# Attention, routed experts and a domain mixture on one core: routing work, meta scatters and first loads put in another order

## The chip, the cores and the metric

The kernel runs on one core of one Trainium2 chip. The metric is the device time of one execution in microseconds (us), as the median of several runs. A profiled execution of the kernel before gives the trace; its clock starts at the first instruction of the program, and all times below count from there. The engines are TensorE (PE, with its weight loads as PEld), VectorE (DVE), ScalarE (ACT), GpSimd (POOL) and SyncE (SP), which only issues transfers. A name with a q behind it (PEldq, SPq) is the engine's own sequencer: register loads, branches and issues of transfers.

## The reference

Three stages in float32, on 2 x 576 = 1152 tokens of 512 features:

```python
# attention: 8 heads of 64; heads 0-3 see the last 32 positions, heads 4-7 every 32nd position
scores = scale * q @ k.T            # masked, softmax, then @ v
x = attn_out.transpose(0, 2, 1, 3).reshape(1152, 512)

# routed experts: one of 8 per token
logits = x @ w_gate + modality_bias[modality_id]
e_idx = argmax(logits, 1); gate_w = softmax(logits)[n, e_idx]
for e in range(8):
    out[mask_e] = gate_w[mask_e, None] * (relu(x[mask_e] @ w1[e]) @ w2[e])   # 512 -> 1024 -> 512

# mixture of 4 domains: every token through every domain
p = domain_probs / domain_probs.sum(-1)
for e in range(4):
    out += p[:, e:e+1] * (relu(x @ u1[e]) @ u2[e])
```

## The kernel before, in words

Every engine has its own program, written out by hand, and they meet at semaphores. There is no planner: the order of the instructions in each program is the order of the work, and a wait stops all that stands behind it on that engine.

**Attention** (TensorE from line 1258, VectorE from 862, ScalarE from 583, GpSimd from 468, all over the same step number i). There are STEPS = 22 blocks of queries, 11 for each of the 2 batches (5 of the strided heads, then 6 of 96 rows of the local heads). In step i TensorE makes the scores of block i, transposes the probabilities of block i - 3 and multiplies block i - 5 with v; VectorE finds row maxima and reciprocal sums and copies results to xT; ScalarE does the exponentials; GpSimd multiplies with the reciprocal (line 471). When enough blocks are done, a token tile (128 tokens, NT = 9 of them) is flipped to rows (flip_rows) and kept in xtok by ScalarE (even tiles) or VectorE (odd tiles), and its 8 logits are computed (gate_logits).

**Routing** is done in three groups of three token tiles. find_experts (line 795) makes the one-hot choice of a group, rank_group on TensorE (1245) counts the tokens before each one, find_slots (814) turns that into a row number in the buffer x_by_expert in device memory, in which each expert has a range of rows. After the first group, at CHOSEN_AT = block 13 (step 18), choose_first (821) picks the expert with the most tokens so far, so that its weights and its first two tiles can be worked on before all is known. put_in_order (831) gives its start rows x_first (columns 0 and 1: first and second tile, 3: the tail to be filled with zeros) and the order of the other experts; find_bases (849) prepares the table of tiles. All three are small instructions on VectorE inside attention steps: choose_first in step 18, put_in_order and the find_slots of the first group in step 19, find_bases in step 20.

**Scatter** (465). GpSimd writes each token tile's rows to x_by_expert with one indirect transfer per tile. The first tile is scattered behind the product of step 20, the second and third after the loop, the other six when the first expert tile has been loaded (xt_in) and their slots are known.

**SyncE's queue** (from 336) is one list: inputs; w1 of the first expert once first_known; a zero fill behind the expert's rows; the first tile x_tile (375) once the fill and the first three scatters have landed; w2 of that expert (376); fill and second tile (381, 385); eight more fills (389); the third tile (394); then a loop that loads w1 and w2 of the other experts; last the sorted meta rows (409).

**Expert tiles.** Float32 products are made of three products of parts in float32r (hi x hi, hi x lo, lo x hi). ScalarE rounds the high part (cut_w1, cut_w2, keep_xt, keep_ht), VectorE subtracts for the low part (split_w1, split_w2, keep_xt, keep_ht). One tile on TensorE (whole_tile, 1382): 24 matmuls of 128x512 with w1 in two halves, flips of h, x and y between them, 24 matmuls with w2. w1 comes in four chunks; the first expert's are cut and split in steps W1_AT = 23 to 26 of the attention loop. Tiles 0 and 1 are written out (1392 to 1409), the others run in a loop whose bounds each engine loads from the table (1412 to 1416 on TensorE, 1097 to 1105 on VectorE). The table comes from count_tiles, find_offsets, make_table and place_tiles on VectorE (984 to 1060), and signals table_ready.

**Meta.** find_meta (1062) gives each token its rank in the sorted order, and a row with its number, and its gate weight times the four domain probabilities. Nine indirect transfers of GpSimd (489), one per token tile, sort these rows into meta_by_rank; the mixture reads them. After them GpSimd waits for the y of the third tile and loads and splits the first domain weights.

**Mixture** (from 1421). All tokens, sorted, go through the four domains; half of the steps use a seven-product scheme for 2x2 blocks. Results are added up in acc and scattered to out. The diff does not touch it.

Of the kernel before, what the change touches and what calls it, by code (L numbers as in the profile page):

```python
# [22 lines left out]
ALU = mybir.AluOpType  # L23
# [17 lines left out]
def moe_chain(nc, qT_in, kT_in, v_in_pos, v_in_res, modality_id, w_gate, modality_bias, w1, w2, domain_probs, u1, u2, out):  # L41
# [65 lines left out]
    W1_AT = [STEPS + LAG_V - 4 + c for c in range(4)]  # L107
# [40 lines left out]
    with ctx:  # L148
# [188 lines left out]
        def _(sp):  # L337
# [12 lines left out]
            for b in range(B):  # L350
                if b == 1:
                    sp.wait_ge(kT_zeroed_g, 1)
                for kind, tiles in ((0, range(STRIDED)), (1, range(STRIDED, TILES))):
                    load_qk(b, kind)
                    for n in tiles:
# [12 lines left out]
            sp.wait_ge(x_first_known, 1)  # L368
# [7 lines left out]
            sp.dma_start(w2_raw[:].unsqueeze(1),  # L376
                         w2[bass.ds(expert, 1)].rearrange("e (c p) d -> p e c d", p=P)).then_inc(w2_in, 16)
# [7 lines left out]
            sp.dma_start(x_tile[:], xb[bass.ds(x1, P), :]).then_inc(xt_in, 16)  # L385
            sp.wait_ge(rest_known, 1)
# [3 lines left out]
            sp.wait_ge(x2_known, 1)  # L390
            x2 = sp.value_load(x_first[0:1, 2:3], min_val=0, max_val=(E - 1) * ROWS + 2 * P)
            sp.wait_ge(filled, 16 * E)
            sp.wait_ge(xt_flipped, 2)
            sp.dma_start(x_tile[:], xb[bass.ds(x2, P), :]).then_inc(xt_in, 16)
# [18 lines left out]
        def _(pool):  # L413
# [54 lines left out]
            for i in range(STEPS):  # L468
                R, C, s = rows(i % TILES), keys(i % TILES), i % PB
                pool.wait_ge(inv_known, i + 1)  # L470
                g.tensor_tensor(prob[0:R, s, :, 0:C], prob[0:R, s, :, 0:C],
                                row_inv[0:R, s, :].unsqueeze(2).to_broadcast([R, HALF_H, C]),
                                ALU.mult).then_inc(normed, 1)
                if i == STEPS - 2:
                    pool.wait_ge(slot_ready, 1)
                    pool.wait_ge(x_kept_a, 2)
                    pool.wait_ge(x_kept_v, 1)
                    scatter(0)
            for t in range(1, NT):
                for g_, (t0, t1) in enumerate(GROUPS):  # L480
                    if t == t0:
                        pool.wait_ge(xt_in, 16)
                        pool.wait_ge(slot_ready, g_ + 1)
                        pool.wait_ge(x_kept_a, (t1 + 1) // 2)
                        pool.wait_ge(x_kept_v, t1 // 2)
                scatter(t)
            pool.wait_ge(meta_ready, 3)
            for t in range(NT):
                pool.indirect_dma_start(out=ms, out_offset=bass.IndirectOffsetOnAxis(ap=pos[:, t:t + 1], axis=0),
                                        in_=meta[:, t, :], in_offset=None).then_inc(meta_scattered, 16)  # L490
            pool.wait_ge(scattered, 16 * (NT - GROUPS[0][1]))
# [48 lines left out]
            pool.wait_ge(y_kept, 3)  # L540
# [3 lines left out]
            split_u2(0)  # L544

# [27 lines left out]
        def _(act):  # L573
# [62 lines left out]
            for t in FLIP_END:  # L636
                if t % 2 == 0:
                    keep_rows(t)
            act.wait_ge(w2_in, 16)
# [16 lines left out]
            keep_xt(2)  # L656
            act.wait_ge(table_ready, 1)
            act.wait_ge(filled, 16 * E)
            load_x(3)
            keep_ht(1, 1)  # L660
# [91 lines left out]
        def _(dve):  # L752
# [37 lines left out]
            def step(ins):  # L790

                ins.then_inc(vstep, 1)
                dve.wait_ge(vstep, st.next())
# [27 lines left out]
            def choose_first():  # L821

                dve.wait_ge(vstep, st.value)
                step(w.reduce_max(choice[:, 0:1], count_a[:], axis=AX.X))
                step(w.scalar_tensor_tensor(out=early_n[:], in0=count_a[:], scalar=choice[:, 0:1], in1=e_down[:],
                                            op0=ALU.is_ge, op1=ALU.mult))
                step(w.reduce_max(choice[:, 1:2], early_n[:], axis=AX.X))
                w.tensor_scalar(first_expert[:], choice[:, 1:2], -1.0, float(E), ALU.mult, ALU.add).then_inc(first_known, 1)
                step(w.tensor_scalar(is_e0[:], e_down[:], choice[:, 1:2], None, ALU.is_equal))

            def put_in_order():
# [4 lines left out]
                w.tensor_copy(x_first[:, 0:1], choice[:, 2:3]).then_inc(vstep, 1)  # L836
                st.next()
                w.tensor_tensor(x_first[:, 3:4], choice[:, 2:3], choice[:, 0:1], ALU.add).then_inc(vstep, 1)
                st.next()
                step(w.tensor_tensor(x_first[:, 1:2], choice[:, 2:3], choice[:, 3:4], ALU.add))  # L840
                w.tensor_scalar(at_least[:], is_e0[:], float(EARLY), None, ALU.mult).then_inc(x_first_known, 1)
# [20 lines left out]
            for i in range(STEPS + LAG_V):  # L862
# [60 lines left out]
                if m == CHOSEN_AT + 1:  # L923
                    put_in_order()
                    find_slots(slice(*GROUPS[0]))
                if m == CHOSEN_AT + 2:
                    find_bases()
# [15 lines left out]
            keep_xt(0)  # L943
            dve.wait_ge(logit_done, 1)
# [149 lines left out]
            keep_y(1)  # L1094
# [3 lines left out]
            n_runs = dve.value_load(table[0:1, 4, 0:1], min_val=1, max_val=E)  # L1098
            with dve.Fori(0, n_runs) as r:
# [126 lines left out]
        def _(pe):  # L1226
# [174 lines left out]
            x_w1(0, 0, 0, range(DC)).then_inc(h_done, 1)  # L1401
            rank_last()
            x_w1(0, 0, 1, range(DC // 2))
# [150 lines left out]
```

## Time and profile before

| what | value |
|---|---|
| median of 3 runs | 650.02 us (649.83 to 651.19) |
| the profiled execution's own time | 652.64 us |
| its span, first to last instruction | 650.9 us |
| TensorE busy | 614.7 us, 94% |
| VectorE / ScalarE / GpSimd busy | 55% / 32% / 46% |
| mean granted clock of TensorE | 0.967 |
| chain that ended last: TensorE | 84% |
| chain: VectorE / issue / transfers / ScalarE / unknown queue | 6% / 4% / 2% / 1% / 1% |

The page cuts the span in 40 slices of 16.3 us. TensorE's granted clock, in tenths, is 9 (full) in all of them but the six slices from 49 to 146 us, where it is 8, 5, 8, 7, 8 and 7. Attention runs to about 76 us, the expert tiles from 81 to 265 us, the mixture from there to the end. How to read it: busy shares are averages over stages with different limits, so what an edit is worth is read from the chain and the waits of the stage it lies in. Ends of matmuls are modelled. In a timeline row the columns are start, duration, engine, line, operation, output and inputs, and in brackets how long the engine had been idle and what released it. A chain row has start, duration and the engine and line that the end of the program waited for at that time.

### The profile page before, as it was taken

Reading aid. Unit: us, or ns where it says so; the run is one execution under the profiler, and the core shown is the slowest. Engines: PE = TensorE matmul, PEld = TensorE weight load, DVE = VectorE, ACT = ScalarE, POOL = GpSimd, SP = SyncE. Lnnn points to the kernel's source line nnn. Section 1 sums busy time; section 2 is a strip of 40 time slices with the busy share of each in tenths; the row PEclk is TensorE's granted clock in tenths of the full one; section 3 lists DMA queues with packets and bytes.
Section 4 is the critical chain, followed back from the end, with each engine's and each line's share of the span. In section 5 each row is a group of like instructions: output and inputs, shape, how many; then the busy total and the mean of one; then the engine's idle time right before and its main releaser. Section 6 shows DMA issues by size and latency. Waiting matters only on the chain.

```text
span 650.9 us, 10557 instructions
## 1 busy us (share of the span) xinstructions
PE 614.7 (94%) x3604; PEld 536.9 (82%) x3605; DVE 358.5 (55%) x735; ACT 207.7 (32%) x528; POOL 299.6 (46%) x278
## 2 busy tenths in 40 slices
PE   5998988969999999999999999999999999999995
PEld 4887966758666688989989988988998998998894
DVE  4877655212788722359555455556545545545553
ACT  3865332212777423204213212311321321231230
POOL 6534230335000000571999685485576568547005
PEclk9998587879999999999999999999999999999999
DMA  9904533723478400100122201110110110110003
GB/s 234 230 3 157 201 125 134 277 52 109 161 274 281 139 16 16 49 33 1 64 65 66 65 33 33 66 51 14 64 64 5 59 64 32 32 64 0 0 0 146
DMA packets 27091, 56.68 MB, mean 87 GB/s; under 512 B 6840, under 2 KB 9528, under 8 KB 27064
## 3 DMA queue, kind: packets, MB, share of 16 engines
q1 hardware_dynamic: 18632, 31.93, 15.4%
q0 software_dynamic: 6848, 21.52, 9.7%
q10 hardware_dynamic: 1584, 2.88, 1.6%
q8 instruction: 15, 0.25, 0.2%
q14 instruction: 12, 0.10, 0.1%
HBM read 48.97 MB, written 7.36 MB: 87 GB/s over the span
## 4 chain that ended last, share of the span: by engine, by line
PE 84%; DVE 6%; issue 4%; DMA 2%; ACT 1%; another core or an unknown queue 1%; POOL 1%; ACTq 0%; SPq 0%; DVEq 0%; POOLq 0%
PE bank L1456 30%; PE bank L1427 28%; PE bank L1351 9%; PE bank L1363 6%; PE bank L1276 2%; PE bank L1242 2%; PE bank L1313 1%; DVE w_lo L859 1%; PE bank L1341 1%; PE bank L1237 1%; PE bank L1286 1%; DMA kT<-in_kT 1%; PE bank L1335 1%; PE bank L1271 1%
## 5 line engine op out<-in xcount | busy, mean ns | idle before, releaser
L1148 DVE SCALAR_TENSOR_TENSOR acc<-bank,meta_s,acc 128x512 f32<-128x512 f32 x135 | 100.8, 749 | 63.3 <-PE bank L1456 63.2
L1456 PE MATMUL bank<-u_hi,h_hi 128*128 128x512 f32 x288 | 112.3, 390 | 0.0
L1456 PE MATMUL bank<-u_lo,h_hi 128*128 128x512 f32 x288 | 112.1, 389 | 0.0
L1456 PE MATMUL bank<-u_hi,h_lo 128*128 128x512 f32 x288 | 112.0, 389 | 0.0
L516 POOL CAST u_hi<-u_raw 128x1792 fp32r<-128x1792 f32 (+1 forms) x16 | 25.6, 1600 | 112.3 <-PE bank L1427 110.0
L1195 DVE SCALAR_TENSOR_TENSOR h_lo<-bank,h_hi 128x288 fp32r<-128x288 f32 x112 | 51.0, 455 | 44.7 <-ACT h_hi L728 22.9
L1427 PE MATMUL bank<-x2T_hi,u_hi 128*128 128x288 f32 x232 | 68.4, 295 | 0.0
L1427 PE MATMUL bank<-x2T_lo,u_hi 128*128 128x288 f32 x232 | 68.4, 295 | 0.0
L1427 PE MATMUL bank<-x2T_hi,u_lo 128*128 128x288 f32 x232 | 68.3, 295 | 0.0
L1427 PE MATMUL bank<-t_hi,u_hi 128*128 128x288 f32 x224 | 66.2, 295 | 0.0
L1427 PE MATMUL bank<-t_lo,u_hi 128*128 128x288 f32 x224 | 66.0, 295 | 0.0
L1427 PE MATMUL bank<-t_hi,u_lo 128*128 128x288 f32 x224 | 65.9, 294 | 0.0
L1456 PEld LDWEIGHTS bank<-u_hi,h_lo 128*128 128x128 f32 x288 | 54.1, 188 | 11.4
L1456 PEld LDWEIGHTS bank<-u_hi,h_hi 128*128 128x128 f32 x288 | 54.0, 188 | 10.2
L1456 PEld LDWEIGHTS bank<-u_lo,h_hi 128*128 128x128 f32 x288 | 54.1, 188 | 10.1
L518 POOL TENSOR_TENSOR u_lo<-u_raw,u_hi 128x1792 fp32r<-128x1792 f32 (+1 forms) x16 | 61.6, 3850 | 1.3
L716 ACT COPY part_p<-bank 128x288 f32<-128x288 f32 x28 | 11.2, 401 | 157.9 <-PE bank L1427 157.9
L508 POOL TENSOR_TENSOR u_raw<-u_raw 128x256 f32<-128x256 f32 x14 | 10.3, 736 | 88.1 <-PE bank L1427 71.4
L1351 PE MATMUL bank<-w_hi,xt_hi 128*128 128x512 f32 x96 | 42.5, 443 | 4.7 <-DVE w_lo L859 3.0
L1427 PEld LDWEIGHTS bank<-x2T_hi,u_hi 128*128 128x128 f32 x232 | 43.5, 188 | 0.7
L1427 PEld LDWEIGHTS bank<-x2T_lo,u_hi 128*128 128x128 f32 x232 | 43.5, 188 | 0.6
L1427 PEld LDWEIGHTS bank<-x2T_hi,u_lo 128*128 128x128 f32 x232 | 43.5, 188 | 0.0
(226 smaller groups left out, 1258.8 us busy)
## 6 DMA issues: line engine op xcount, KB each, us to landing
w_raw<-in_moe_w SPq DMA_DIRECT2D x10, 2048.0 KB, 8.9
u_raw<-in_moe_w POOLq DMA_DIRECT2D x16, 512.0 KB, 3.7
u_raw<-in_moe_w POOLq DMA_DIRECT2D x16, 256.0 KB, 3.1
u_raw<-in_moe_w POOLq DMA_DIRECT2D x32, 128.0 KB, 2.9
x_tile<-x_by_expert ACTq DMA_DIRECT2D x11, 256.0 KB
x_by_expert<-zero_row SPq DMA_DIRECT2D x10, 256.0 KB, 2.0
qT<-in_qT SPq DMA_DIRECT2D x4, 576.0 KB, 8.4
kT<-in_kT SPq DMA_DIRECT2D x8, 288.0 KB, 9.7
```

The lines of the kernel that those rows point to most:

```text
L508: g.tensor_tensor(u1_raw[:, S1], u1_raw[:, A21], u1_raw[:, A22], ALU.add).then_inc(u_summed, 1)
L516: g.tensor_copy(u1_hi[n % 2][:, need], u1_raw[:, need]).then_inc(u1_hi_cut, 1)
L518: g.tensor_tensor(u1_lo[n % 2][:, need], u1_raw[:, need], u1_hi[n % 2][:, need].bitcast(FP32), ALU.subtract)\
L716: a.copy(part[s][k][:], bank[s][:, 0:SUB]).then_inc(part_kept[s], 1)
L1148: w.scalar_tensor_tensor(out=acc[:, t, :], in0=bank[Z_BANK[i]][:], scalar=meta_s[:, t, bass.ds(e + 1, 1)], in1=acc[:, t, :], op0=ALU.mult, ...
L1195: w.scalar_tensor_tensor(out=h_lo[:, i, cols_of(s, k)], in0=bank[at][:, 0:SUB], scalar=0.0, in1=h_hi[:, i, cols_of(s, k)].bitcast(FP32), o ...
L1242: last = t_.matmul(where, xT[:, c, P * t:P * (t + 1)], gate[:, c, :], start=c == 0, stop=c == DC - 1)
L1276: last = t_.matmul(bank_s[0:R, h, 0:C], qT[:, b, c, q0:q0 + R], kT[:, b, c, h % 2, k0:k0 + C], start=False, stop=True, skip_group_check=True)
L1351: last = t_.matmul(bank[half][:], lhs[:, c, :], rhs[:, c, fs], start=c == 0 and i == 0, stop=c == DC - 1 and i == 2)
L1363: last = t_.matmul(bank[5][:], lhs[:, f, :], rhs[:, f, :], start=f == 0 and rhs is w2_hi and lhs is ht_hi, stop=f == FCH - 1 and lhs is ht_lo)
L1427: last = t_.matmul(bank[at][:, 0:SUB], lhs_part[page][:, lhs, c, :], rhs[:, c, :], start=start and c == 0 and i == 0, stop=c == KC - 1 and ...
L1456: last = t_.matmul(bank[Z_BANK[i]][:], lhs[:, c, ts], rhs[page][:, c, :], start=c == 0 and k == 0, stop=c == 1 and k == 2)
```

## The change

- **Spread.** The rows x_first are made by a new function place_first, one attention step after choose_first; find_slots of the first group comes one step later than before (step 20), the rest of put_in_order in step 21, find_bases in step 22.
- **Scatters.** The first three scatters are issued behind the products of steps 19, 20 and 21.
- **First loads.** SyncE issues the w2 load as soon as x_first is known, before the zero fill and the first tile. The third tile's load is put before the eight fills and no longer waits for them.
- **w1 chunks.** Three chunks are cut and split in steps 24 to 26; the fourth after the loop (ScalarE: behind its last row copy; VectorE: behind keep_xt(0), ahead of the last logits). TensorE's rank_last moves between the third and the fourth chunk of the first product.
- **Waits before the loop.** ScalarE does keep_ht(1, 1) before it waits for the table and the fills. VectorE does keep_y(1) after find_meta and after its loads of n_tiles and n_runs.
- **Meta.** The scatter of meta block t waits for y of tile t; the first three stand before the loads and splits of the first domain weights, the other six behind them.

```diff
-    W1_AT = [STEPS + LAG_V - 4 + c for c in range(4)]
+    SCATTER_FROM = STEPS - GROUPS[0][1]
+    W1_AT = [STEPS + LAG_V - 3 + c for c in range(3)]
```

On SyncE:

```diff
-            sp.wait_ge(x_first_known, 1)
+            sp.wait_ge(x_first_known, 3)
+            sp.dma_start(w2_raw[:].unsqueeze(1),
+                         w2[bass.ds(expert, 1)].rearrange("e (c p) d -> p e c d", p=P)).then_inc(w2_in, 16)
             x0 = sp.value_load(x_first[0:1, 0:1], min_val=0, max_val=(E - 1) * ROWS)
...
             sp.dma_start(x_tile[:], xb[bass.ds(x0, P), :]).then_inc(xt_in, 16)
-            sp.dma_start(w2_raw[:].unsqueeze(1),
-                         w2[bass.ds(expert, 1)].rearrange("e (c p) d -> p e c d", p=P)).then_inc(w2_in, 16)
...
+            sp.wait_ge(x2_known, 1)
+            x2 = sp.value_load(x_first[0:1, 2:3], min_val=0, max_val=(E - 1) * ROWS + 2 * P)
+            sp.wait_ge(xt_flipped, 2)
+            sp.dma_start(x_tile[:], xb[bass.ds(x2, P), :]).then_inc(xt_in, 16)
             sp.wait_ge(rest_known, 1)
             for e in range(E):
                 tail = sp.value_load(fill_rest[0:1, e:e + 1], min_val=0, max_val=E * ROWS)
                 sp.dma_start(xb[bass.ds(tail, P), :], zero_row[:]).then_inc(filled, 16)
-            sp.wait_ge(x2_known, 1)
-            x2 = sp.value_load(x_first[0:1, 2:3], min_val=0, max_val=(E - 1) * ROWS + 2 * P)
-            sp.wait_ge(filled, 16 * E)
-            sp.wait_ge(xt_flipped, 2)
-            sp.dma_start(x_tile[:], xb[bass.ds(x2, P), :]).then_inc(xt_in, 16)
```

On GpSimd (the issue of one meta block is as before):

```diff
-                if i == STEPS - 2:
+                if i == SCATTER_FROM:
                     pool.wait_ge(slot_ready, 1)
                     pool.wait_ge(x_kept_a, 2)
                     pool.wait_ge(x_kept_v, 1)
-                    scatter(0)
-            for t in range(1, NT):
+                if i >= SCATTER_FROM:
+                    scatter(i - SCATTER_FROM)
+            for t in range(GROUPS[0][1], NT):
...
-            pool.wait_ge(meta_ready, 3)
-            for t in range(NT):
+            def scatter_meta(t):
+                pool.wait_ge(y_kept, t + 1)
                 pool.indirect_dma_start(out=ms, out_offset=bass.IndirectOffsetOnAxis(ap=pos[:, t:t + 1], axis=0),
...
-            pool.wait_ge(y_kept, 3)
+            pool.wait_ge(meta_ready, 3)
+            for t in range(3):
+                scatter_meta(t)
             load_u1(0)
             load_u2(0)
             split_u1(0)
             split_u2(0)
+            for t in range(3, NT):
+                scatter_meta(t)
```

On ScalarE:

```diff
                     keep_rows(t)
+            cut_w1(WCH - 1)
             act.wait_ge(w2_in, 16)
...
             keep_xt(2)
+            keep_ht(1, 1)
             act.wait_ge(table_ready, 1)
             act.wait_ge(filled, 16 * E)
             load_x(3)
-            keep_ht(1, 1)
```

On VectorE:

```diff
+            def place_first():

                 w.tensor_scalar(choice[:, 2:3], choice[:, 1:2], -float(ROWS), float(E * ROWS), ALU.mult, ALU.add).then_inc(vstep, 1)
                 st.next()
                 step(w.tensor_scalar(choice[:, 3:4], choice[:, 0:1], float(P), None, ALU.min))
-                w.tensor_copy(x_first[:, 0:1], choice[:, 2:3]).then_inc(vstep, 1)
+                w.tensor_copy(x_first[:, 0:1], choice[:, 2:3]).then_inc(x_first_known, 1)
+                w.tensor_tensor(x_first[:, 3:4], choice[:, 2:3], choice[:, 0:1], ALU.add).then_inc(x_first_known, 1)
+                w.tensor_tensor(x_first[:, 1:2], choice[:, 2:3], choice[:, 3:4], ALU.add).then_inc(x_first_known, 1)
+
             def put_in_order():
+                step(w.tensor_scalar(is_e0[:], e_down[:], choice[:, 1:2], None, ALU.is_equal))
...
                 if m == CHOSEN_AT + 1:
+                    place_first()
+                if m == CHOSEN_AT + 2:
+                    find_slots(slice(*GROUPS[0]))
+                if m == CHOSEN_AT + 3:
                     put_in_order()
-                    find_slots(slice(*GROUPS[0]))
-                if m == CHOSEN_AT + 2:
+                if m == CHOSEN_AT + 4:
                     find_bases()
...
             keep_xt(0)
+            split_w1(0, WCH - 1)
             dve.wait_ge(logit_done, 1)
...
-            keep_y(1)
             find_meta()
             dve.wait_ge(table_ready, 1)
             n_tiles = dve.value_load(table[0:1, 4, 1:2], min_val=EARLY + 1, max_val=MAXT)
             n_runs = dve.value_load(table[0:1, 4, 0:1], min_val=1, max_val=E)
+            keep_y(1)
```

On TensorE:

```diff
-            x_w1(0, 0, 0, range(DC)).then_inc(h_done, 1)
+            x_w1(0, 0, 0, range(DC - 1))
             rank_last()
+            x_w1(0, 0, 0, range(DC - 1, DC)).then_inc(h_done, 1)
```

## Rows read from the trace of the kernel before

**Rows 1.** Timeline of TensorE: start, us, engine, line, operation, idle before

```profile
60.32 0.55 PE L1286 MATMUL bank<-ident,prob 96*128 96x96 f32 x4 [2.19 <-POOL prob L471]
...
115.18 1.48 PE L1363 MATMUL bank<-w_hi,ht_hi 128*128 128x512 f32 x4 [2.45 <-ACT ht_hi L623]
...
136.05 2.08 PE L1363 MATMUL bank<-w_hi,ht_hi 128*128 128x512 f32 x4 [5.70 <-ACT ht_hi L623]
```

**Rows 2.** Timelines of VectorE and ScalarE, routing work and the end of attention

```profile
55.65 0.16 DVE L833 TENSOR_SCALAR choice<-choice 128x1 f32<-128x1 f32 x1
...
57.91 0.17 DVE L819 CAST slot<-slot_f 128x3 uint32<-128x3 f32 x1
...
80.11 0.17 DVE L946 TENSOR_TENSOR logits<-bank,bias_tok 128x16 f32<-128x16 f32 x1 [1.56 <-PE bank L1242]
...
81.18 0.18 DVE L805 TENSOR_TENSOR onehot<-r,first 128x24 bf16<-128x24 f32 x1
...
81.53 1.99 ACT L611 CAST w_hi<-w_raw 128x1024 fp32r<-128x1024 f32 x2
...
86.03 0.18 DVE L810 TENSOR_TENSOR rank_e<-bank,e_rows 128x24 f32<-128x24 f32 x1 [4.52 <-PE bank L1249]
...
113.08 0.68 DVE L938 TENSOR_TENSOR xt_lo<-bank,xt_hi 128x512 fp32r<-128x512 f32 x1
```

**Rows 3.** Windows: length, busy PE, PEld, DVE, ACT, POOL, PEclk, DMA share, GB/s

```profile
61.30:85.00 23.70, 22.61 (x122) 20.72 (x121) 12.73 (x39) 10.00 (x19) 8.10 (x8) 0.50 0.54 196
...
115.90:119.30 3.40, 3.40 (x10) 2.62 (x9) 0.00 (x0) 0.00 (x0) 0.00 (x0) 0.50 0.97 344
...
132.90:139.80 6.90, 3.75 (x9) 2.98 (x10) 0.69 (x1) 0.59 (x1) 0.67 (x1) 0.51 0.01 1
```

**Rows 4.** Chain of waits in order of time: start, us, what was waited for

```profile
76.00 0.85 PE bank L1329 x4
...
81.02 4.75 PE bank L1351 x12
...
94.95 2.51 DMA x_tile<-x_by_expert
...
99.56 5.49 PE bank L1351 x12
...
119.78 2.74 PE bank L1351 x12
...
128.10 7.29 another core or an unknown queue
...
140.81 2.75 PE bank L1351 x12
...
153.62 2.72 PE bank L1351 x12
```

**Rows 5.** Timeline of SyncE's queue, the first expert's loads

```profile
54.96 0.39 SPq L366 DMA_DIRECT2D w_raw<-in_moe_w  x1
...
58.03 0.38 SPq L372 DMA_DIRECT2D x_by_expert<-zero_row  x1
...
69.67 0.36 SPq L375 DMA_DIRECT2D x_tile<-x_by_expert  x1
```

**Rows 6.** Two weight loads in a row: window 114 to 129, queue 1 from 122.4

```profile
114.00:129.00 15.00, 13.72 (x60) 10.99 (x60) 4.11 (x13) 3.47 (x6) 4.96 (x6) 0.89 0.81 298
...
q1 hardware_dynamic: 763, 1.58, 103.2%
```

**Rows 7.** Register loads from the table on TensorE and VectorE, by line

```profile
L1412 PEldq TENSOR_LOAD <-table x1: 488/488/488, 115.9 to 115.9; - x1
...
L1100 DVEq TENSOR_LOAD <-table x5: 302/307/324, 123.7 to 213.1; - x5
L1097 DVEq TENSOR_LOAD <-table x1: 553/553/553, 122.0 to 122.0; - x1
```

**Rows 8.** Transfers into meta_by_rank: ns min, median, max, first and last start

```profile
L489 POOL DMA_INDIRECT meta_by_rank<-meta,pos x9: 952/957/961, 122.5 to 132.6; - x9
```

More of the change, by code:

```diff
@@ L828, in choose_first @@
                 w.tensor_scalar(first_expert[:], choice[:, 1:2], -1.0, float(E), ALU.mult, ALU.add).then_inc(first_known, 1)
-                step(w.tensor_scalar(is_e0[:], e_down[:], choice[:, 1:2], None, ALU.is_equal))
-            def put_in_order():
+            def place_first():
                 w.tensor_scalar(choice[:, 2:3], choice[:, 1:2], -float(ROWS), float(E * ROWS), ALU.mult, ALU.add).then_inc(vstep, 1)
@@ L835, in put_in_order @@
                 step(w.tensor_scalar(choice[:, 3:4], choice[:, 0:1], float(P), None, ALU.min))
-                w.tensor_copy(x_first[:, 0:1], choice[:, 2:3]).then_inc(vstep, 1)
+                w.tensor_copy(x_first[:, 0:1], choice[:, 2:3]).then_inc(x_first_known, 1)
+                w.tensor_tensor(x_first[:, 3:4], choice[:, 2:3], choice[:, 0:1], ALU.add).then_inc(x_first_known, 1)
+                w.tensor_tensor(x_first[:, 1:2], choice[:, 2:3], choice[:, 3:4], ALU.add).then_inc(x_first_known, 1)
+            def put_in_order():
+                step(w.tensor_scalar(is_e0[:], e_down[:], choice[:, 1:2], None, ALU.is_equal))
+                w.tensor_scalar(at_least[:], is_e0[:], float(EARLY), None, ALU.mult).then_inc(vstep, 1)
                 st.next()
[L838 to L841, printed above, removed]
                 w.tensor_scalar(early_n[:], is_e0[:], choice[:, 3:4], None, ALU.mult).then_inc(vstep, 1)
```

## Prediction

> **What bounds the kernel now.** I read the granted clock by stretch first, then the chain of waits in order of time from 45 to 170 us, then the timelines of the engines where that chain leaves TensorE. From 139.8 us on the chain is TensorE's almost alone and the page's clock line shows full speed; the diff touches nothing there except some of the meta scatters. So the change can only win before that point, by letting the later work start earlier. Between 61 and 140 us the reader should see four losses. (a) TensorE waits 2.19 us for GpSimd's softmax product at 60.32 [rows 1], which waits for VectorE's routing work [rows 2], and the clock is at half (1.2 of 2.4 GHz) from 61.3 to 85 us [rows 3]. (b) It idles until the second token tile lands (94.95 + 2.51 us) and then runs 12 matmuls in 5.49 us that take 2.74 us at full clock [rows 4]. (c) It waits 2.45 us for ScalarE's ht_hi at 115.18 [rows 1], which stands behind the wait for the table on ScalarE; the clock is at half again [rows 3]. (d) It waits 5.70 us at 136.05 [rows 1]: the chain has 7.29 us of "another core or an unknown queue" just before [rows 4].
>
> **First part: routing work, scatters and the first loads.** put_in_order and find_slots are 13 small VectorE instructions from 55.65 to 58.08 [rows 2], in one attention step. After the change that step keeps only the five of place_first (0.9 us), find_slots goes to the next step, the rest to the two after. The product that TensorE waited for at 60.32 comes some 1.8 us earlier. The three scatters issue at about 59 to 65 us, between products, instead of from 63; each holds GpSimd some 1.2 us, which delays the products of the last two steps by 0.3 and 0.7 us.
>
> That is not worth 1.8 us, because of what is late next: the first token tile. SyncE now issues the w2 load right behind w1, ahead of the zero fill (issued at 58.03) and of the tile load (69.67) [rows 5]. I take one queue to serve them in order (no row shows the fill's landing), and the tile load waits for the fill. w1 and w2 (2.1 MB each), the fill and three scatters (0.26 MB each) are 5.2 MB. When w1 and w2 went back to back they moved at 298 GB/s over their whole stretch and at 1.58 MB in 4 us, 395 GB/s, in its middle [rows 6]; so they need 13 to 17.5 us from 54.96, to 68.3 to 72.4. I take 72.0, near the slow end, since that row includes start and tail. The tile then reaches TensorE after 2.5 us more [rows 4], at 74.5. Before, TensorE came to it at 76.00 without a wait. Gain 1.5 us. The slow end gives 1.1, or 0 if TensorE's own work is late; the fast end puts the tile at 70.8, where TensorE's own work would set the time, 3 us earlier at most.
>
> From there the order is by hand. Tile flip, 16 logit matmuls and row flip take 5.0 us (76.00 to 81.02), so x_w1 starts at 79.5. The fourth chunk of w1 is now cut by ScalarE after its last row copy (0.6 us; a cut is half of the 1.99 us at 81.53 [rows 2]; so 81.1), VectorE splits it (1.2 us: 82.3), and only then takes the last logits and finds the experts (80.11 to 81.36, 1.25 us [rows 2]): 83.6. That work had been ready 4 us before it was needed, and is now just on time: TensorE reaches rank_last after 9 instead of 12 of the half-clock matmuls (3.6 instead of 4.75 us), at 83.1, waits 0.5 us and is done at 83.9. VectorE's rank_e was at 86.03; it moves up 2.1 us, and with it the last three scatters, the second tile's load and x_w1 of tile 1. **Term 1: -2.1 us.** Bounds 0 and -3.5. The cover of the moved split_w1 is thin: each microsecond by which it is late is lost whole.
>
> Asking for the third tile before the eight fills moves a load that TensorE did not wait for; the fills then end about 107 us by their 1 us pace, before the table. I cost it at nothing; without that cover ScalarE's next tile load would wait for them.
>
> **Second part: the wait on ScalarE.** keep_ht(1,1) now precedes the table wait. ScalarE's half can be ready at 112.4. VectorE places tiles to 113.2, then xt_lo (113.08 + 0.68 [rows 2]) and ht_lo end at 114.45, and TensorE's matmuls at 115.4 instead of 119.6. But TensorE's own register loads of the table start only once ht_lo is known: the first is at 115.9 [rows 7], and the first matmul of tile 2 is at 119.62, 3.6 us later. That chain is not removed. It starts at 114.5, so tile 2 starts at 118.1. **Term 2: -1.5 us**, not the 4.2 us by which the matmuls of tile 1 end earlier. The gap left, 115.4 to 118.1, is 2.7 us. Gaps of 2.19, 2.45 and 5.70 us were each followed by half clock [rows 1, 3], 3.4 us of it after the gap of 2.45. Before, that stretch lay on the last matmuls of tile 1; now it lies on tile 2. **Term 3: +1.7 us** (half of 3.4), bounds 0 and +3.4.
>
> keep_y(1) now stands behind find_meta (1.8 us) and two register loads: the next one begins at 123.7 [rows 7], 1.7 us after the first of these two at 121.96. VectorE gets to it at 117.6 and is done at 118.3; TensorE wants y after the first 12 matmuls of tile 2, at 120.8. Nothing; without that cover, 2.2 us.
>
> **Third part: the meta rows.** Nine scatters were issued from 122.5 to 133.6 us [rows 8], one each 1.26 us. Now two go out near 116 us, the third when y of tile 2 is kept, then one per tile. In tile 2 TensorE takes from 119.78 to 140.81 us; tile 3 takes 12.81 us [rows 4]. The excess of 8.2 us is the 5.70 us wait and the half clock behind it. The semaphore of a flip that ran at 128.3 is seen by ScalarE at 135.4, and the nine scatters are what is peculiar to this stretch: the six weight loads of the later runs come without it. If the burst is the cause, it is gone. **Term 4: -8.2 us.** It is a guess at a cause which the trace does not name; bounds 0 and -8.2.
>
> The page "DMA: Bandwidth & Descriptors" of the Trainium skill, section "Queues, rings and completion order", says that each DMA engine takes turns between the rings with work, a packet at a time. By it four scatters issued from 122.5 would have been served among the weight packets and no burst could pile up. The trace disagrees so far: from 122.4 to 126.4 us four were issued and queue 1 alone moved packets, 763 of them [rows 6].
>
> **Sum.** -2.1 - 1.5 + 1.7 - 8.2 = -10.1 us against the profiled execution's 652.64 us: 642.5. Its span is 650.9, 1.7 us lies around it, and it is 2.6 us above the median of 650.02. For the median I subtract the same: 639.9 us.
>
> **Rivals.**
> *The stall of tile 2 is not the burst's* but belongs to the weight loads and ends with them. For it: it comes as 4.2 MB drain, and the rule above would have it so. Against: the loads are over some 7 us before it ends. The stall then stays and moves with table_ready: -2.1, and -1.5 + 1.7 as above, in sum -1.9, so 648.1; or -5 (645.0) where the clock does not fall. Chance 0.33.
> *The clock holds in tile 1 as well.* The second tile comes 2.1 us earlier and tile 0 ends only 1 us earlier, so the idle time before its flip shrinks by 1 us; that from the flip to x_w1 (97.46 to 99.56 [rows 4]) stays. Then x_w1 of tile 1 takes 2.74 for 5.49 us, and term 3 may fall away: 639.9 - 2.75 - 1.7 = 635.4. Chance 0.15.
> *The first part is no gain.* The tile comes at 76, behind w2, or the late split_w1 eats it: 639.9 + 2.1 = 642.0. Chance 0.1 beside the forecast. It is also the case in which the spreading does not do what it says.
> *Slower: scattered meta rows stop many tiles.* If one scatter is enough to hold TensorE's semaphore, the seven that now go one per tile each cost up to 8.2 us where nothing stood before; for it speaks only that the cause is unknown. With term 4 still gained, two tiles give 639.9 + 16.4 = 656.3. It decides from two tiles on. Chance 0.07.
> The forecast has 0.35.
>
> **Numbers.** 0.2% is 1.3 us, about what a measurement of this kernel can tell from no change. Gains of all cases but the last are above it, save the lower half of the first rival (bound +3.4 in term 3 makes it -0.2): 0.09 go to no change. Faster 0.83, same 0.09, slower 0.08. Range 635.0 (the clock rival) to 648.5 (the first rival at its point, with 0.4 for its bound).
>
> **What would show it.** Right: no 2.2 us wait for GpSimd near 60; x_tile's first load after w2 in the queue and TensorE idle before the flip; rank_e near 84; ht_hi of tile 1 right behind its flip, then a gap of some 2.7 us that ends with the register loads; tile 2 near 13 to 15 us; meta scatters one per tile. Wrong: a wait of several microseconds in tile 2 (first rival), w2 on the chain in front of x_tile by over 2 us, or VectorE's split_w1 on the chain before rank_last; GpSimd's meta in front of stalls in tiles 3 to 9.

## The result, and the profile after

The changed kernel takes 640.39 us (median of 4 runs, 639.28 to 640.56), the kernel before 649.92 us beside it (median of 4, 648.67 to 651.19): ratio 0.985, 95% interval 0.9827 to 0.9872. The forecast was 639.9 us. The profiled executions are 652.64 and 640.29 us, 12.35 apart. That is 2.8 us more than the medians are, because the profiled execution before lies 2.7 us above its median.

The page after has TensorE busy for 609.7 us of a span of 638.5, mean granted clock 0.978 (before 0.967). Its clock line, 40 slices of 16 us:

```profile
PEclk9999588899999999999999999999999999999999
```

TensorE's timeline after, at the places of the change (columns as in [rows 1]):

```profile
58.34 0.55 PE L1299 MATMUL bank<-ident,prob 96*128 96x96 f32 x4 [0.38 <-POOL prob L471]
...
74.52 1.12 PE L1342 MATMUL bank<-ident,x_tile 128*128 128x128 f32 x4 [1.83 <-DMA x_tile<-x_by_expert]
...
83.84 0.20 PE L1259 MATMUL bank<-onehot,before 128*128 128x24 bf16 x1 [0.21 <-DVE onehot L812]
...
95.87 0.66 PE L1342 MATMUL bank<-ident,x_tile 128*128 128x128 f32 x4 [1.31 <-DMA x_tile<-x_by_expert]
```

The wait of 2.19 us for GpSimd's product [rows 1] is 0.38 us. Now TensorE waits 1.83 us for the first tile's transfer, where before it came to it without a wait (76.00, [rows 4]). VectorE around the moved split_w1:

```profile
81.39 1.23 DVE L868 TENSOR_TENSOR w_lo<-w_raw,w_hi 128x1024 fp32r<-128x1024 f32 x1 [4.41 <-ACT w_hi L582]
82.54 0.17 DVE L959 TENSOR_TENSOR logits<-bank,bias_tok 128x16 f32<-128x16 f32 x1
...
84.29 0.18 DVE L817 TENSOR_TENSOR rank_e<-bank,e_rows 128x24 f32<-128x24 f32 x1 [0.36 <-PE bank L1262]
```

rank_e is 1.7 us earlier than at 86.03 [rows 2]. The chain after (columns as in [rows 4]; "x12" are the first twelve matmuls of a tile):

```profile
57.82 14.11 DMA x_by_expert<-zero_row
72.10 2.37 DMA x_tile<-x_by_expert
...
97.93 4.59 PE bank L1364 x12
...
112.73 2.29 issue
115.02 4.61 PE bank L1364 x12
...
129.71 2.72 PE bank L1364 x12
```

Against [rows 4]: tile 1 starts at 97.93 for 99.56, tile 2 at 115.02 (119.78 on that chain, 119.62 with its first matmul), tile 3 at 129.71 for 140.81. The row of 7.29 us of an unknown queue has no successor. Tile 2 takes 14.7 us instead of 21.0. Tile 3 starts 11.1 us earlier, and nearly all of this stays: the mixture's first product on the chain is at 254.44 for 265.31 us, 10.9 us earlier. The last 1.5 us of the 12.35 come at the very end. TensorE's last 48 matmuls run alike in both (their first and last starts are 10.66 us apart), but VectorE's last addition waits 0.61 us for TensorE where it waited 1.72 us before:

```profile
644.55 0.75 DVE L1148 SCALAR_TENSOR_TENSOR acc<-bank,meta_s,acc 128x512 f32<-128x512 f32 x1 [1.72 <-PE bank L1456]
632.58 0.75 DVE L1161 SCALAR_TENSOR_TENSOR acc<-bank,meta_s,acc 128x512 f32<-128x512 f32 x1 [0.61 <-PE bank L1470]
```

The first row is of the kernel before. The change touches nothing there, so these 1.5 us are not shown to be its work. The zero fill, which [rows 4] did not show landing, now lands 14.11 us after its issue, behind w1 and w2 in the queue. Half clock is left from 64.2 to 84.7, 98.3 to 101.7 and 115.4 to 118.8:

```profile
64.20:84.70 20.50, 18.04 (x109) 15.68 (x108) 11.22 (x33) 7.29 (x9) 3.61 (x4) 0.50 0.46 176
98.30:101.70 3.40, 3.40 (x10) 2.64 (x9) 2.93 (x17) 0.00 (x0) 0.00 (x0) 0.51 0.73 280
115.40:118.80 3.40, 3.40 (x10) 2.65 (x9) 0.00 (x0) 0.00 (x0) 0.95 (x1) 0.51 1.02 408
119.00:140.00 21.00, 21.00 (x109) 17.24 (x108) 6.07 (x9) 6.72 (x12) 6.47 (x7) 1.00 0.57 177
```

The columns are those of [rows 3]. The last row is full clock from 119 to 140, where before 5.70 us of waiting and 6.9 us of half clock lay.

### The profile page after: what moved, and what is told of

It reads as the page before. It is cut to its first block, busy times and chain, and to the rows that moved or that the text cites. A ratio compares the mean times of both kernels' runs of the same rounds, so it can differ in the third digit from the quotient of the medians.

```text
span 638.5 us, 10555 instructions
## 1 busy us (share of the span) xinstructions
PE 609.7 (95%) x3604; PEld 531.9 (83%) x3605; DVE 359.8 (56%) x735; ACT 207.2 (32%) x528; POOL 300.1 (47%) x278
## 3 DMA queue, kind: packets, MB, share of 16 engines
q0 software_dynamic: 6848, 21.52, 10.1%
## 4 chain that ended last, share of the span: by engine, by line
PE 82%; DMA 6%; issue 4%; DVE 4%; POOL 2%; ACT 2%; SPq 0%; DVEq 0%; ACTq 0%; POOLq 0%
PE bank L1470 29%; PE bank L1441 28%; PE bank L1364 8%; PE bank L1376 6%; PE bank L1289 3%; DMA x_by_expert<-zero_row 2%; DMA w_raw<-in_moe_w 1%; POOL out L573 1%; DVE w_lo L868 1%; PE bank L1354 1%; PE bank L1326 1%; PE bank L1299 1%; PE bank L1255 1%; PE bank L1284 1%; DMA kT<-in_kT 1%
## 5 line engine op out<-in xcount | busy, mean ns | idle before, releaser
L1470 PEld LDWEIGHTS bank<-u_hi,h_hi 128*128 128x128 f32 x288 | 54.0, 188 | 10.1
L1470 PEld LDWEIGHTS bank<-u_lo,h_hi 128*128 128x128 f32 x288 | 54.1, 188 | 10.1
L490 POOL DMA_INDIRECT meta_by_rank<-meta,pos x9 | 8.8, 976 | 102.1 <-DVE y_tile L995 78.7
## 6 DMA issues: line engine op xcount, KB each, us to landing
kT<-in_kT SPq DMA_DIRECT2D x8, 288.0 KB, 10.1
```

The lines of the kernel that those rows point to most:

```text
L1470: last = t_.matmul(bank[Z_BANK[i]][:], lhs[:, c, ts], rhs[page][:, c, :], start=c == 0 and k == 0, stop=c == 1 and k == 2)
```

## The experiments

The experiments ran in three sets (1 to 4, 5 to 8, 9 to 12), each with the kernel before beside it: medians 650.66, 650.83 and 650.39 us. "The changed kernel" stands below for 640.39 us, measured beside 649.92 us. The median of one kernel moves by up to 0.9 us from set to set, so a difference of that size between sets says nothing.

**1. The changed kernel with the burst back.**

```diff
-                pool.wait_ge(y_kept, t + 1)
-            for t in range(3):
+            for t in range(NT):
                 scatter_meta(t)
+            pool.wait_ge(y_kept, 3)
             load_u1(0)
...
-            for t in range(3, NT):
-                scatter_meta(t)
```

> The changed kernel (640.4 us), with all nine meta scatters issued together again as soon as the meta rows are ready, all else as changed. If the burst made the 5.70 us wait in tile 2 of the kernel before, the wait comes back: tile 2 takes about 8 us more than its 14.7 us (115.02 to 129.71), and the kernel takes 646 to 649 us. If the wait belonged to the weight loads or to something else that the other edits removed, tile 2 stays within 0.5 us and the kernel at 640.4 +/- 0.8 us. If the wait is shorter in most runs than in the one profiled (which was 2.7 us above the median), 642 to 646 us.

643.68 us (642.8 to 643.99, 5 runs), ratio 0.9896, interval 0.9875 to 0.9917: 3.3 us above the changed kernel. The unknown queue is back on the chain in tile 2:

```profile
115.24 4.56 PE bank L1362 x12
...
120.93 3.18 another core or an unknown queue
...
124.44 2.54 another core or an unknown queue
...
132.06 2.72 PE bank L1362 x12
```

Tile 2 takes 16.8 us for 14.7, and not the 8 us more that were expected. The scatters start at 114.20, before tile 2, so they are over sooner within it: ScalarE's two waits cost TensorE waits of 0.90 and 0.78 us, and its clock stays up.

**2. The kernel before with the meta scatters spread,** and nothing else of the change.

```diff
-            pool.wait_ge(meta_ready, 3)
-            for t in range(NT):
+            def scatter_meta(t):
+                pool.wait_ge(y_kept, t + 1)
...
-            pool.wait_ge(y_kept, 3)
+            pool.wait_ge(meta_ready, 3)
+            for t in range(3):
+                scatter_meta(t)
             load_u1(0)
...
+            for t in range(3, NT):
+                scatter_meta(t)
```

> The kernel before (649.9 us), with the meta scatters alone spread as in the change: three before the first domain weights, six behind, each behind the y of its tile. If the burst is the cause: about 8.2 us less in tile 2 (128.10 to 135.39 on the chain gone), 641.7 us, or some 644 if the wait is shorter in most runs. If the weight loads are the cause: the wait is there at the same place and the time is 649.9 +/- 0.8 us.

643.69 us (642.49 to 645.04, 6 runs), ratio 0.9899, interval 0.9878 to 0.9919: 7.0 us below the kernel before. Its waits from 110 to 136 us, all of them:

```profile
114.57 1.77 PE L1367 MATMUL bank<-w_hi,ht_hi 128*128 128x512 f32 x4 [2.29 <-ACT ht_hi L627]
128.54 1.21 PE L1367 MATMUL bank<-w_hi,ht_lo 128*128 128x512 f32 x4 [0.24 <-DVE ht_lo L975]
```

The 5.70 us are gone, and tile 3 starts at 132.50 for 140.81. The third part alone is therefore worth 7.0 us on the kernel before, and 3.3 us with the other parts in place.

**3. The changed kernel with ScalarE's wait back.**

```diff
-            keep_ht(1, 1)
             act.wait_ge(table_ready, 1)
             act.wait_ge(filled, 16 * E)
             load_x(3)
+            keep_ht(1, 1)
```

> The changed kernel, with ScalarE's keep_ht(1,1) behind the table wait, the fills and the tile load again. By the prediction's term 2: ht_hi of tile 1 at about 111.7 instead of 108.9, TensorE's first matmul of tile 2 some 1.5 us later (116.5 instead of 115.0) because its register loads start behind ht_lo; the half clock stretch then lies on the last matmuls of tile 1 instead of tile 2, which gives back up to 1.7 us: 640.2 to 641.9 us. A rival that counts the whole ScalarE wait says 2.7 us or more: 643 us.

640.64 us (639.12 to 644.48, 6 runs), ratio 0.9858, interval 0.983 to 0.9886: no different from the changed kernel. TensorE's wait splits in two as before, and the sum is larger:

```profile
115.07 1.20 PE L1376 MATMUL bank<-w_hi,ht_hi 128*128 128x512 f32 x4 [2.45 <-ACT ht_hi L629]
119.28 0.49 PE L1364 MATMUL bank<-w_hi,xt_hi 128*128 128x512 f32 x1 [1.17 <-issue]
```

3.62 us of waiting against 2.29 us. But tile 1's first twelve matmuls ran at full clock here (3.03 us from 102.27) and tile 2 began 17.0 us after them; in the changed kernel it was 17.1 us with 1.6 us of half clock in it. The edit is worth some 1.5 us at equal clock, and no median shows it.

**4. w2 behind the first tile again.**

```diff
-            sp.dma_start(w2_raw[:].unsqueeze(1), ...).then_inc(w2_in, 16)
             x0 = sp.value_load(x_first[0:1, 0:1], min_val=0, max_val=(E - 1) * ROWS)
...
             sp.dma_start(x_tile[:], xb[bass.ds(x0, P), :]).then_inc(xt_in, 16)
+            sp.dma_start(w2_raw[:].unsqueeze(1), ...).then_inc(w2_in, 16)
```

> The changed kernel, with the first w2 load behind the first token tile's load again, as before. If the fill stands behind w2 in the queue (58 to 71.9 us on the chain), the fill lands near 64, the tile near 69.5 to 70, and TensorE flips it when it comes to it, at 72.7 instead of 74.5: 1.8 us less down the chain, 638.6 us, with w2 landing near 78, just before ScalarE cuts it at 79.5. If the scatters set the tile's arrival and not w2, the flip stays at 74.5 and the time at 640.4. If w2 then comes late at ScalarE or TensorE, over 640.4.

638.47 us (637.62 to 644.25, 6 runs), ratio 0.982, interval 0.9798 to 0.9843: 1.9 us below the changed kernel, with an interval that overlaps that kernel's by a little (0.9827 to 0.9872). The wait of 1.83 us for x_tile before the first flip is gone. That alone proves little, since the profiled execution, 644.25 us, is 5.8 above the median and reaches the flip only at 80.05 us. Run 10 has the same edit in an undisturbed execution: there the tile's load goes out at 67.91 us (72.10 in the changed kernel), and the flip at 73.74 waits for nothing. The tile's load in run 10, then in the changed kernel:

```profile
67.91 0.37 SPq L376 DMA_DIRECT2D x_tile<-x_by_expert  x1
72.10 0.36 SPq L378 DMA_DIRECT2D x_tile<-x_by_expert  x1
```

So w2 ahead made the first tile late; that this cost 1.9 us is likely and not clear of noise.

**5. The rank product earlier.** rank_last after the first chunk of the first product instead of the third; VectorE splits the fourth chunk of w1 and computes lexp only after the slots of the last group.

```diff
-            x_w1(0, 0, 0, range(DC - 1))
+            x_w1(0, 0, 0, range(1))
             rank_last()
-            x_w1(0, 0, 0, range(DC - 1, DC)).then_inc(h_done, 1)
+            x_w1(0, 0, 0, range(1, DC)).then_inc(h_done, 1)
...
-            split_w1(0, WCH - 1)
...
-            w.tensor_tensor(lexp[:], logits[:], lmax[:].unsqueeze(2).to_broadcast([P, NT, E]), ALU.subtract)\
-             .then_inc(lmax_known, 1)
...
             find_slots(slice(*GROUPS[2]))
+            split_w1(0, WCH - 1)
...
+            w.tensor_tensor(lexp[:], logits[:], lmax[:].unsqueeze(2).to_broadcast([P, NT, E]), ALU.subtract)\
+             .then_inc(lmax_known, 1)
             split_w2(0, 0)
```

> The changed kernel, with rank_last behind the first chunk of x_w1 instead of the third, and VectorE's split of the fourth w1 chunk behind the last slots instead of ahead of the last logits. Theory: the moved split held back the last experts (82.54 to 83.84) and TensorE's rank was placed for it. rank_e moves from 84.29 to about 81.6, the second tile's load from 93.2 to 90.5, so its 1.31 us wait (95.87) goes and the chain is TensorE's own work up to the flip: 1.3 us less, 639.1 us, up to 1.5 us more if the clock does not fall there. If the last scatters are not what the second tile waits for, 640.4.

636.87 us (634.86 to 639.01, 6 runs), ratio 0.979, interval 0.9766 to 0.9814: 3.5 us better, where 1.3 us were expected, or up to 2.8 if the clock did not fall. rank_e is at 81.70 for 84.29, the second tile's flip waits for no transfer, and tile 1 starts here:

```profile
96.37 0.50 PE L1364 MATMUL bank<-w_hi,xt_hi 128*128 128x512 f32 x1 [1.40 <-DVE xt_lo L950]
```

The chain from the rank over the scatters to the second tile was what still bound this stage. Not all of the 3.5 us can be put down to it: the first twelve matmuls of tile 1 take 3.02 us here for 4.59, and run 12 shows that this 1.6 us can come without any edit. Against the profiled execution of run 12, which also held its clock there, tile 1 starts 2.7 us earlier (96.37 for 99.09).

**6. TensorE's register loads earlier.** It loads n_runs and n_tiles before its last wait for ht_lo of tile 1, not behind tile 1.

```diff
+                extra = before_last() if before_last else None
                 pe.wait_ge(ht_kept, j * NHALF + 2)
                 h_w2(r, second, ht_lo, w2_hi).then_inc(y_done, 1)
+                return extra
...
-            whole_tile(1, 0)
-            pe.wait_ge(table_ready, 1)
-            n_runs = ...
-            n_tiles = ...
+            n_runs, n_tiles = whole_tile(1, 0, load_counts)
```

(load_counts holds the three lines that are taken out.)

> The changed kernel, with TensorE's two register loads of n_runs and n_tiles ahead of its wait for ht_lo of tile 1 instead of behind the tile. Theory (term 2): the gap before tile 2 (2.29 us at 115.02) is the four register loads that start when ht_lo is known (111.5); two of them can run from 110.3, when the table is ready, so the last four matmuls of tile 1 start up to 0.5 us later and tile 2 about 1.1 us earlier: 639.3 us, up to 1.7 us less if the shorter gap keeps the clock up. If the gap is something else, no change: 640.4.

638.15 us (637.3 to 639.39, 5 runs), ratio 0.9802, interval 0.9783 to 0.9821: 2.2 us better. The chain's row for the gap is 0.88 us instead of 2.29:

```profile
98.62 4.61 PE bank L1364 x12
...
113.73 0.88 issue
114.61 3.01 PE bank L1364 x12
```

So the gap was the register loads', as the prediction had it. The full clock behind it is no proof of the edit: see run 12.

**7. The burst later.** All nine meta scatters in a row, but behind y of tile 5.

```diff
-                pool.wait_ge(y_kept, t + 1)
-            for t in range(3):
-                scatter_meta(t)
+            pool.wait_ge(y_kept, 3)
             load_u1(0)
...
-            for t in range(3, NT):
+            pool.wait_ge(y_kept, 5)
+            for t in range(NT):
                 scatter_meta(t)
```

> The changed kernel, with all nine meta scatters in a row behind the y of the fifth tile, when no weights are being loaded. If nine in a row hold TensorE's semaphores by themselves, waits with an unknown releaser appear in that tile, and the time is 642.5 to 644 us as with the burst at its old place (643.7). If the burst hurts only while weights load, nothing shows and the time is 640.4 us.

642.03 us (640.09 to 645.15, 5 runs), ratio 0.9877, interval 0.985 to 0.9903, which overlaps that of the changed kernel; whether the 1.6 us are real is open. The trace is clear. The expectation took it that no weights would be loading then, but the next expert's were: the nine scatters run among 3.34 MB of weight loads (window 157 to 173, queues), and no row of an unknown queue stands on the chain from 145 to 185 us; the longest wait of TensorE from 150 to 180 us is the last row:

```profile
q1 hardware_dynamic: 1133, 3.34, 64.1%
q10 hardware_dynamic: 144, 0.26, 11.2%
q0 software_dynamic: 215, 0.02, 1.0%
```

```profile
169.75 0.49 PE L1363 MATMUL bank<-w_hi,xt_hi 128*128 128x512 f32 x1 [1.00 <-DVE w_lo L867]
```

A burst is not enough by itself; it has to fall at a certain place.

**8. The routing work in its old steps,** the rest of the change kept.

```diff
                 if m == CHOSEN_AT + 1:
                     place_first()
-                if m == CHOSEN_AT + 2:
-                    find_slots(slice(*GROUPS[0]))
-                if m == CHOSEN_AT + 3:
                     put_in_order()
-                if m == CHOSEN_AT + 4:
+                    find_slots(slice(*GROUPS[0]))
+                if m == CHOSEN_AT + 2:
                     find_bases()
```

> The changed kernel, with all routing work of VectorE in the two attention steps where it was (place_first, put_in_order and find_slots in step 19, find_bases in step 20). By the prediction the spreading is hidden: the first token tile, which waits for the fill behind w2, comes at 74.5 either way, so 640.4 +/- 0.8 us, with TensorE's wait for GpSimd (2.2 us) back near 58. A rival that takes the spreading for the gain says 642 us or more.

641.03 us (639.69 to 644.18, 6 runs), ratio 0.9865, interval 0.9838 to 0.9891: no different. The wait of [rows 1] returns, and tile 2 still starts at 114.95 (115.02):

```profile
60.46 0.90 PE L1297 MATMUL bank<-ident,prob 96*128 96x96 f32 x4 [2.09 <-POOL prob L471]
```

With w2 ahead of the first tile, the spreading is hidden by the wait for that tile.

**9. Both: w2 behind the tile and the routing unspread.** The edits of 4 and 8 together.

> The kernel of e4 (w2 behind the first tile's load, 638.5 us) with the routing work in the two attention steps where it was. There the first tile no longer sets the time of its flip, TensorE's own work does, so the spreading should now count: about 1.5 to 2 us more, 640 to 640.5 us. If it stays at 638.5, the spreading is worth nothing even when the tile is early.

642.18 us (639.09 to 642.99, 6 runs), ratio 0.9867, interval 0.9841 to 0.9894: 3.7 us above run 4, in another set. The direction is as expected, since with the tile early nothing covers the 2.08 us at 60.10. The size is not to be trusted: the runs fall in two heaps, 639 to 640 and 642 to 643, and against run 12 of its own set it is 1.0 us.

**10. Runs 4, 5 and 6 in one kernel.** The three edits as shown.

> The changed kernel with the edits of e4 (w2 behind the first tile), e5 (rank early, -3.5 us) and e6 (register loads early, -2.2 us) together. If they add up with e4's -1.9: 632.8 us. What e5 and e6 gained beyond their waits was clock that stayed up, which may be had only once, and e4's earlier flip may be lost again at the last scatters: then 634 to 636 us. Over 636.9 would mean that they get in each other's way, w2 arriving too late being the first suspect.

632.56 us (630.87 to 641.12, 6 runs), ratio 0.9723, interval 0.9697 to 0.9749. The single gains of 1.9, 3.5 and 2.2 us add up to 7.6; it lies 7.8 us below the changed kernel, 8.6 below run 12 of its set, and 17.8 below the kernel before. Five of its six runs lie between 630.87 and 633.89 us. Its chain around tile 2, and its clock line:

```profile
94.26 3.02 PE bank L1364 x12
...
107.79 0.88 issue
108.67 2.99 PE bank L1364 x12
...
121.74 2.72 PE bank L1364 x12
```

```profile
PEclk9999599999999999999999999999999999999999
```

Only one slice is left below 9.

**11. The kernel before, without weight loads during the burst.** SyncE loads the next experts' weights only when all nine meta scatters have landed.

```diff
+            sp.wait_ge(meta_scattered, 16 * NT)
             with sp.If(n_runs > 1):
```

> The kernel before, with SyncE's loop of weight loads for the other experts held until all nine meta scatters have landed (134.6 us instead of 114.7; the weights are wanted at 163). The burst keeps its place and meets no weight load. If burst and loads together make the wait in tile 2: gone, 642 to 644 us as with the meta rows spread. If the burst does it alone: the wait stays, 650 us. More than 650 if the later loads come too late for the second expert.

651.2 us (649.53 to 651.61, 12 runs), ratio 1.0009, interval 0.9992 to 1.0025. The loads now go out at 134.43, so nothing of queue 1 moves in the stretch. The wait stays, on the chain and on TensorE:

```profile
126.75 7.20 another core or an unknown queue
```

```profile
134.61 2.07 PE L1364 MATMUL bank<-w_hi,ht_hi 128*128 128x512 f32 x4 [5.57 <-ACT ht_hi L624]
```

Together with run 7 this rules the weight loads out from both sides: this burst stalls ScalarE without them, and a later burst among them does not.

**12. The changed kernel once more,** unchanged, as a yardstick for 9 and 10.

> The changed kernel as it is, beside the others of this call: 640.4 us, with the first token tile flipped at about 74.5, a gap of 2.3 us before tile 2 and no wait in tile 2. Every theory expects the same; the run is the yardstick for differences of 1 us.

641.15 us (638.64 to 642.22, 6 runs), ratio 0.9855, interval 0.983 to 0.9879. Its profiled execution, 638.64 us, holds full clock where the other one of the same kernel did not:

```profile
99.09 3.02 PE bank L1364 x12
...
112.29 2.30 issue
114.59 3.03 PE bank L1364 x12
...
127.69 2.72 PE bank L1364 x12
```

4.59 and 4.61 us there, 3.02 and 3.03 us here, behind gaps of 2.29 and 2.30 us. Tile 3 starts 2.0 us earlier although tile 1 started 1.2 us later. So 3 us of clock come and go between executions of one kernel.

## Why the prediction was right

The time was right, 639.9 against 640.39 us, and of the steps most held in size.

**First part (term 1, -2.1 us).** The flip was put at 74.5 and came at 74.52, with the tile's landing as what ends the wait. Split_w1 was put at 81.1 to 82.3 and ran from 81.39 to 82.62; rank_e, put at 83.9, came at 84.29. So 1.7 us were gained, and tile 1 starts 1.6 us earlier. That w2 in front takes back most of what the spreading brings was right: run 8 shows the spreading worth nothing with w2 in front, and runs 4 and 10 show the tile arriving earlier without it. The thin cover of split_w1 was named, and run 5, which moves split_w1 and the rank together, is 3.5 us better.

**Second part (term 2, -1.5; term 3, +1.7).** The gap before tile 2 was put at 2.7 us and is 2.29, run 6 shows it to be the register loads', and the half-clock stretch moved onto tile 2 as said (115.4 to 118.8). Term 2 is confirmed at equal clock by run 3, and its sum with term 3, forecast at +0.2 us, by run 3's median, 0.25 us above the changed kernel. What the steps missed is in tile 1: its first product took 4.59 us, not 5.49, because less of it lay at half clock. That is 0.9 of the 1.0 us by which tile 2 starts ahead of the 116.0 that the steps give (118.1 less 2.1).

**Third part (term 4, -8.2 us).** The burst is the cause: runs 1 and 2 put it in and take it out, and the wait comes and goes with it. Tile 2 was to become 6.5 us shorter by terms 3 and 4 and became 6.3 (21.0 to 14.7). In medians the burst is worth 7.0 us on the kernel before and 3.3 on the changed one. So 8.2 us is the size in one profiled execution of the kernel before, 2.7 us above the median, and not what the edit brings where the scatters start before tile 2. The other two parts bring 3.3 us once the burst is spread (run 2 against the changed kernel), where the sum of terms 1 to 3 was 1.9. The two errors have opposite signs, and some of the closeness of the forecast is owed to that.

**The last step was luck.** For a profiled execution the sum gave 642.5 us (652.64 less 10.1), and it took 640.29: 12.35 us came off. That is 2.25 us more than the sum: 1.0 us is there when tile 3 starts, nearly all of it tile 1's clock, 0.2 us is lost again before the mixture, and 1.5 us comes at the program's end. The forecast then took off 2.6 us more, on the assumption that the changed kernel's profiled execution would also lie above its median. It lay 0.1 us below it. The two misses cancel, and in medians 9.5 us came off where the sum said 10.1.

**The rivals.** That the stall belongs to the weight loads (0.33) has fallen, by run 11. The DMA page of the Trainium skill ("DMA: Bandwidth & Descriptors", section "Queues, rings and completion order") says that a DMA engine takes turns between its rings. The prediction said that the trace disagreed so far, and its window ended too soon: in the kernel before, queue 0 moves 51 packets beside 168 of queue 1 from 126.4 to 127.4 us. In run 1 the two queues move together as well while the weights drain, from 121 to 122 us:

```profile
q1 hardware_dynamic: 130, 0.26, 78.5%
q0 software_dynamic: 27, 0.00, 4.5%
q14 instruction: 1, 0.01, 2.8%
```

These rows agree with the page's rule; they say nothing on the stall, which needs no queue 1 at all. That the clock holds in tile 1 as well (0.15) came true in part: not in the profiled execution of the result, but in that of run 12. That the first part is no gain (0.1) is wrong: rank_e is 1.7 us and tile 1 is 1.6 us earlier. The slower rival (0.07), that one scatter is enough to stop a tile, is wrong: the seven that stand alone leave no wait of an unknown queue, and even nine in a row leave none in run 7.

**What stays open** is what the burst holds up. In all three executions with the stall it ends 1.7 to 1.8 us after GpSimd has issued the last of the nine: 132.29 to 133.95 us in run 11, 125.24 to 126.98 in run 1, 133.6 to 135.4 in the kernel before. In all three a transfer that the profile calls "instruction" starts within 0.9 us of its start (queue 14: at 125.97, 121.37 and 127.29 us); in run 11, from 125.5 to 128 us, it is the middle row:

```profile
q10 hardware_dynamic: 19, 0.04, 26.8%
q14 instruction: 1, 0.01, 3.8%
q0 software_dynamic: 32, 0.00, 2.2%
```

Neither of the two is enough alone. In run 7 the burst starts at 157.42 us, and the last transfer of queue 14 ahead of it is at 151.85: no stall. In run 2 such a transfer is at 126.86 us, with two scatters before it and none in the 6 us after it: no stall either, and the same holds for the changed kernel, where it is at 121.07. This would fit an engine, ScalarE by the chain, which waits for the next piece of its program while small indirect transfers are being issued. It would also fit a signal from TensorE that is held up only at the loop's first pass. No run parted these two, so neither is shown.

## What to carry to other kernels

Small indirect transfers that nobody waits for are best spread out: nine in a row, at one place of this program, kept another engine waiting for 7 us although they moved hardly any data. When a stage is full of short waits, follow the one that ends last and ask what is late next: here a spread of VectorE's work brought nothing because a transfer put in front of the tile had become the bound, and taking that one, the rank product and the register loads together brought another 7.8 us. Where a gap may or may not cost the clock, one profiled execution does not give the size of an edit; two executions of the same kernel differed by 3 us in it.

## What was not expected of the hardware

- A burst of nine indirect transfers, some 0.96 us of issue each, kept ScalarE waiting for 7.20 us with the DMA engines less than a quarter busy: from 128 to 134 us in run 11 they moved 0.24 MB, nearly all of it one tile load.
- Equal gaps do not give an equal clock: 2.29 and 2.30 us before tile 2 were followed by 4.61 and 3.03 us for the same twelve matmuls. With the gap at 0.88 us both executions seen ran them in 2.99 to 3.01 us.
- Some executions are late already in attention: the product at 58.34 us starts at 64.27 in the profiled execution of run 4, whose 644.25 us are 5.8 above its own median. The profiled execution of run 3 (644.44 us, 3.8 above) is of the same kind. In both the chain has a row of 7.9 to 8.0 us for the transfer of the domain probabilities from about 28.5 us on, TensorE then waits 1.93 and 2.15 us at about 41 us where it waits 0.84 in the changed kernel, and its clock is at half from 40.4 to 50.6 and from 42.3 to 49.1 us, where it is full in the changed kernel. No edit touches this. Only the runs near the median speak of the edit.
